# Attention and two mixture layers: the second layer's turns nested, its last blocks taken by output rows, GpSimd in one scatter loop

## What is computed

```python
logits = x @ w_gate + modality_bias[modality_id]
e_idx = np.argmax(logits, axis=1)
gate_w = softmax(logits)[np.arange(N), e_idx]
for e in range(E):
    mask = e_idx == e
    if not mask.any():
        continue
    h = np.maximum(x[mask] @ w1[e], 0.0)
    out[mask] = gate_w[mask, None] * (h @ w2[e])
```

## Time and profile before

| what | value |
|---|---|
| median of 3 runs | 1515.71 us (1514.54 to 1515.93) |
| the profiled execution's own time | 1515.54 us |
| its span | 1514.0 us |
| its mean granted clock of TensorE | 0.993 |

### The profile page before, as it was taken

How to read it: one execution, slowest core, us unless ns; L and a number is a source line. 1 busy time by engine, 2 the same in 40 slices (tenths; PEclk the granted TensorE clock), 3 DMA queues, 4 the chain that set the end, 5 groups by cost and what they waited for, 6 DMA issues and landing times.

```text
span 1514.0 us, 34658 instructions
## 1 busy us (share of the span) xinstructions
PE 1468.2 (97%) x11861; PEld 1292.1 (85%) x11861; DVE 1011.9 (67%) x2377; ACT 773.6 (51%) x1544; POOL 401.1 (26%) x379
## 2 busy tenths in 40 slices
PE   8999999999999999999899999999999999999994
PEld 7888978789888888788799999998888888888884
DVE  7989977999789998987666666665333333333331
ACT  6676767776677767665344444444333332333331
POOL 4133312334123424212322222224121221221211
PEclk9999999999999999999999999999999999999997
DMA  5311030212202020201533354323211111111110
GB/s 119 98 33 62 28 99 28 65 42 62 79 31 65 28 86 28 85 30 36 170 109 130 129 201 131 104 95 109 73 43 43 44 69 41 42 54 46 42 50 21
DMA packets 58018, 107.86 MB, mean 71 GB/s; under 512 B 18007, under 2 KB 32354, under 8 KB 57884
## 3 DMA queue, kind: packets, MB, share of 16 engines
q0 software_dynamic: 18464, 58.68, 11.1%
q1 hardware_dynamic: 39420, 47.48, 11.1%
HBM read 75.63 MB, written 32.04 MB: 71 GB/s over the span
## 4 chain that ended last, share of the span: by engine, by line
PE 81%; DVE 5%; issue 5%; DMA 4%; ACT 1%; POOL 1%; SPq 0%; POOLq 0%; ACTq 0%; DVEq 0%
PE pO L1436 23%; PE pS L1684 11%; PE pO L1696 10%; PE pS L1644 9%; PE pO L1627 9%; PE pS L1425 6%; PE pO L1698 5%; PE pM L1684 3%; DVE AH L1091 3%; DMA raw<-in_v_dram 2%; DMA token_rows<-xrow,dest 1%; PE pT L1675 1%; PE pT L1574 1%; PE pO L1445 1%; POOL token_rows L527 1%
## 5 line engine op out<-in xcount | busy, mean ns | idle before, releaser
L1093 DVE TENSOR_TENSOR AL<-A,AH 128x512 fp32r<-128x512 f32 (+1 forms) x400 | 314.4, 786 | 13.7
L1436 PE MATMUL pO<-AH,VH 64*128 64x512 f32 (+1 forms) x1520 | 306.7, 384 | 9.2 <-DVE xT L998 7.2
L1436 PE MATMUL pO<-AL,VH 64*128 64x512 f32 (+1 forms) x1520 | 305.4, 382 | 0.0
L1436 PE MATMUL pO<-AH,VL 64*128 64x512 f32 (+1 forms) x1520 | 305.1, 382 | 0.0
L709 ACT ACTIVATE R<-pS 128x512 f32<-128x512 f32 (+1 forms) x400 | 213.5, 588 | 150.4 <-PE pS L1425 134.8
L1091 DVE CAST AH<-A 128x512 fp32r<-128x512 f32 (+1 forms) x400 | 231.7, 579 | 39.8 <-ACT A L718 39.4
L718 ACT ACTIVATE A<-R 128x512 f32<-128x512 f32 (+1 forms) x400 | 229.8, 624 | 19.8 <-DVE AL L1093 19.4
L1696 PE MATMUL pO<-VL,AH 128*128 128x512 f32 x640 | 232.4, 399 | 0.0
L1351 DVE SCALAR_TENSOR_TENSOR AL<-pS,AH 128x512 fp32r<-128x512 f32 x120 | 83.0, 692 | 180.8 <-ACT AH L877 179.3
L1436 PEld LDWEIGHTS pO<-AH,VH 64*128 64x128 f32 x1520 | 154.2, 184 | 34.4 <-issue 12.6
L1698 PE MATMUL pO<-VL,AL 128*128 128x256 f32 x640 | 179.5, 280 | 0.0
(11 more groups left out here) (241 smaller groups left out, 2477.5 us busy)
## 6 DMA issues: line engine op xcount, KB each, us to landing
raw<-in_w_dram POOLq DMA_DIRECT2D x22, 1024.0 KB
A<-token_rows SPq DMA_DIRECT2D x21, 536.0 KB
uT<-in_u_dram SPq DMA_DIRECT2D x16, 512.0 KB
xin<-token_rows SPq DMA_DIRECT2D x24, 268.0 KB
raw<-in_v_dram SPq DMA_DIRECT2D x4, 1152.0 KB, 5.8
A<-in_w2t_dram POOLq DMA_DIRECT2D x8, 512.0 KB
raw<-in_v_dram SPq DMA_DIRECT2D x4, 768.0 KB, 8.1
raw<-in_z_dram SPq DMA_DIRECT2D x8, 368.0 KB
```

The costliest lines, as they stand in the source:

```text
L1093: v_.tensor_tensor(AL[k % NBUF][:, 0:n], A[k % NA][:, 0:n], AH[k % NBUF][:, 0:n].bitcast(F32), ALU.subtract).then_inc(al_ready, 1)
L1436: last = t_.matmul(pO[:, (KD * r + d) * QW:(KD * r + d) * QW + n], vv[rows, vo + k * D + d * P:vo + k * D + (d + 1) * P], a[k % NBUF][rows ...
```

## The change

On TensorE, ScalarE and VectorE the walk over the turns becomes a nest: `turns(at + 1, hi)` stands inside `If(hi < total)` of `turns(at, lo)`, so that behind the last tile one branch leaves all of it. `total` is loaded once by VectorE and TensorE ahead of it. GpSimd has one loop over tiles 1 to `total` with nothing but `scatter_out` in phase 1, and loads one entry of `cum` in place of nine; the work ahead for turns from 1 on goes to VectorE (remainders, `next_low`) and SyncE (the two loads of weights, `load_weights_behind`), both behind `If(hi < total)`. On TensorE `layer1` of block 7 goes ahead of `layer2` of block 4, and blocks 5, 6 and 7 of `layer2` are added row block by row block: all three for s = 0, then for s = 1, and so on (`layer2_last`). In tile 0 the second transpose stands between s = 1 and s = 2.

```diff
+                    def load_weights_behind(turn_):
+
+                        sp.wait_ge(wl_ready, WP * turn_ + 2 * WP)
+                        sp.sem_inc(sp_passed, 1)
+                        e = sp.value_load(order[0:1, turn_ + 2:turn_ + 3], min_val=0, max_val=2 * E - 1)
+                        sp.dma_start(stage1, w1[ds(e, 1), :, :].rearrange("o (k p) f -> p (o k) f", p=P)).then_inc(w1_loaded, 16)
+                        sp.dma_start(stage2, w2[ds(e, 1), :, :].rearrange("o (f p) d -> p (o f) d", p=P)).then_inc(w2_loaded, 16)
...
+                        if ph == 1 and at > 0:
+                            with sp.If(hi < total):
+                                load_weights_behind(at + E)
...
-            for ph in range(2):
-                q = PH[ph]
-                if ph == 1:
-                    next_weights(E, 0, True)
-                    scatter_out(0)
-                pool.wait_ge(cum_ready, ph + 1)
-
-                ends = [pool.value_load(cum[0:1, ph, i:i + 1], min_val=0, max_val=64) for i in range(E + 1)]
-                total = ends[E]
...
-                    turn_ = at + ph * E
-
-                    def ahead():
-                        if ph == 0:
-                            if at + 2 < E:
-                                wait(gcols_made, at + 1)
-                                load_w2t(at + 2)
-                            next_weights(turn_, at % 2, False)
-                        else:
-                            with pool.If(hi < total):
-                                next_weights(turn_, at % 2, True)
-
...
-                            if turn_ != E:
-                                with pool.If(t == lo):
-                                    ahead()
-                            if ph == 1:
-                                scatter_out(t)
-                    if turn_ != E:
-                        with pool.Else():
+            def scatter_rows(t):
...
+            with pool.If(total > 0):
+                scatter_rows(total)
+            next_weights(E, 0, True)
+            scatter_out(0)
+            pool.wait_ge(cum_ready, 2)
+            total = pool.value_load(cum[0:1, 1, E:E + 1], min_val=0, max_val=64)
+            with pool.If(total > 1):
+                with pool.Fori(1, total) as t:
+                    scatter_out(t)
...
-                lo = 1
-                for at in range(E):
+                def turns(at, lo):
+
                     hi = end_of(act, 1, at)
                     turn_, h = at + E, at % 2
...
-                    lo = hi
+                    if at + 1 < E:
+                        with act.If(hi < total):
+                            turns(at + 1, hi)
+
+                turns(0, 1)
                 act.wait_ge(q.stored, STORED + 16 * SUB2 * total)
...
+                total = dve.value_load(cum[0:1, 1, E:E + 1], min_val=0, max_val=64)
+                def turns(at, lo):
+
                     hi = end_of(dve, 1, at)
+
+                    def weights_ahead():
+
+                        with dve.If(hi < total):
+                            next_low(at + E + 1, 1 - at % 2)
...
+                            if at > 0:
+                                with dve.If(t == lo):
+                                    weights_ahead()
...
-                    lo = hi
+                    if at > 0:
+                        with dve.Else():
+                            weights_ahead()
+                    if at + 1 < E:
+                        with dve.If(hi < total):
+                            turns(at + 1, hi)
+
+                turns(0, 1)
...
+                def row_sums(h, f, s):
+
+                    rows = slice(s * P, (s + 1) * P)
+                    t_.matmul(pO[:, s * QW:(s + 1) * QW].rearrange("p (m d) -> p m d", m=2), AH[f][:, rows], w2hl[h][:, :, f, 0:D],
+                              start=(f == 0), stop=(f == NF - 1), skip_group_check=True)
+                    return t_.matmul(pO[:, s * QW:s * QW + D], AL[f][:, rows], w2h[h][:, f, 0:D],
+                                     start=False, stop=(f == NF - 1), skip_group_check=True)
+
                 def layer2(t, h, f):
 
                     pe.wait_ge(q.h_split, NF * t + NF + f + 1)
                     if f == 0:
                         pe.wait_ge(q.y_out, t + 1)
                     for s in range(SUB2):
-                        rows = slice(s * P, (s + 1) * P)
-                        t_.matmul(pO[:, s * QW:(s + 1) * QW].rearrange("p (m d) -> p m d", m=2), AH[f][:, rows], w2hl[h][:, :, f, 0:D],
-                                  start=(f == 0), stop=(f == NF - 1), skip_group_check=True)
-                        last = t_.matmul(pO[:, s * QW:s * QW + D], AL[f][:, rows], w2h[h][:, f, 0:D],
-                                         start=False, stop=(f == NF - 1), skip_group_check=True)
-                        if f == NF - 1:
-                            last.then_inc(q.y_made, 1)
-                    if f < NF - 1:
-                        last.then_inc(q.h_used, 1)
+                        last = row_sums(h, f, s)
+                    last.then_inc(q.h_used, 1)
+
+                def layer2_last(t, h, between=None):
+
+                    for s in range(SUB2):
+                        for f in range(NF - 3, NF):
+                            if s == 0:
+                                pe.wait_ge(q.h_split, NF * t + NF + f + 1)
+                            last = row_sums(h, f, s)
+                            if s == SUB2 - 1 and f < NF - 1:
+                                last.then_inc(q.h_used, 1)
+                        last.then_inc(q.y_made, 1)
+                        if s == 1 and between is not None:
+                            between()
...
-                for f in range(3, NF):
+                for f in range(3, NF - 1):
                     layer2(0, 0, f - 3)
                     layer1(0, 0, 0, f, hring_lead)
+                layer1(0, 0, 0, NF - 1, hring_lead)
+                layer2(0, 0, 4)
                 pe.wait_ge(q.h_split, NF + 6)
                 transpose_half(1, 0, pT)
-                layer2(0, 0, 5)
-                layer2(0, 0, 6)
-                transpose_half(1, 1, pT)
-                layer2(0, 0, 7)
+                layer2_last(0, 0, lambda: transpose_half(1, 1, pT))
                 pe.wait_ge(cum_ready, 2)
-                lo = 1
-                for at in range(E):
+                total = pe.value_load(cum[0:1, 1, E:E + 1], min_val=0, max_val=64)
+
+                def turns(at, lo):
+
                     hi = end_of(pe, 1, at)
                     h = at % 2
                     with pe.If(lo < hi):
@@ -1747,12 +1784,14 @@
                             transpose_half(t + 1, 1, pT)
                             layer2(t, h, 3)
                             layer1(t, par, h, 6, hring)
+                            layer1(t, par, h, 7, hring)
                             layer2(t, h, 4)
-                            layer1(t, par, h, 7, hring)
-                            layer2(t, h, 5)
-                            layer2(t, h, 6)
-                            layer2(t, h, 7)
-                    lo = hi
+                            layer2_last(t, h)
+                    if at + 1 < E:
+                        with pe.If(hi < total):
+                            turns(at + 1, hi)
+
+                turns(0, 1)
```

More of the change, by code:

```diff
@@ L586, in scatter_out @@
                                           bounds_check=N - 1, oob_is_err=False).then_inc(PH[1].stored, 16)
-            for ph in range(2):
-                q = PH[ph]
-                if ph == 1:
-                    next_weights(E, 0, True)
-                    scatter_out(0)
-                pool.wait_ge(cum_ready, ph + 1)
-                ends = [pool.value_load(cum[0:1, ph, i:i + 1], min_val=0, max_val=64) for i in range(E + 1)]
-                total = ends[E]
-                if ph == 0:
[L598 to L602, removed]
-                for at in range(E):
-                    lo, hi = 1 if at + ph * E == E else ends[at], ends[at + 1]
-                    turn_ = at + ph * E
-                    def ahead():
-                        if ph == 0:
-                            if at + 2 < E:
-                                wait(gcols_made, at + 1)
-                                load_w2t(at + 2)
-                            next_weights(turn_, at % 2, False)
-                        else:
-                            with pool.If(hi < total):
-                                next_weights(turn_, at % 2, True)
[L617 to L624, removed]
-                            if turn_ != E:
-                                with pool.If(t == lo):
-                                    ahead()
-                            if ph == 1:
-                                scatter_out(t)
-                    if turn_ != E:
-                        with pool.Else():
-                            ahead()
[L633 to L638, removed]
@@ new lines, in scatter_rows @@
+            def scatter_rows(t):
```

(27 more changed lines are left out.)

## The result

The changed kernel took 1507.49 us (median of 4 runs, 1503.43 to 1508.98) against 1515.82 us for the kernel before: a ratio of 0.9943, 95% interval 0.9922 to 0.9963. Measured again it was 1509.15 against 1515.96, a ratio of 0.9960 (0.9946 to 0.9973). So it is faster by some 7 to 8 us; the forecast was 8.5.

A forecast was written before the change was run, and what follows sets the result against it. TensorE bounds the kernel until the last matmul, then GpSimd's stops and DRAIN. DRAIN start 1498.43 + 6.87 + 0.25 barrier + 1.5 outside the span gives 1507.1, so 1507.2 us for the median; range 1503.0 to 1513.2.

The forecast's parts named there:

- The end is a walk over empty turns and then GpSimd's DRAIN: Behind the last matmul: GpSimd's three stops over empty turns go, so its DRAIN starts 8.5 us sooner, at 1498.43.
- The last scatters, 2.1 us: End of the last tile: row blocks become ready 1.05 us apart, so GpSimd's last scatter ends 2.1 us sooner, at 1498.83.
- The DRAIN as a cost of its own: GpSimd's DRAIN at the end keeps its recorded length of 6.87 us wherever it starts.
- The tied DRAIN: Rival: the end of GpSimd's DRAIN stays 12.9 us behind the last scatter's end, giving 1513.1 us; chance 0.2.
- The short DRAIN: Rival: GpSimd's final DRAIN becomes short and ScalarE's wait for stored rows sets the end, 1503.1 us; chance 0.12.
- Moved weight work, loads of `total`: nothing: Weight work moved to VectorE and SyncE, and register loads on VectorE and TensorE, change the time by nothing.
- Block 7, no stall: TensorE ahead of `layer2` of block 7: 1.88 us needed, 2.1 us covered, 0.2 left; rival of a stall, chance 0.05.
- Tile 0 and 1, 0.4 us less: Second transpose moves 0.7 us forward and `load_x` of tile 2 is issued sooner: 0.4 us taken as gain.
- The new order costs nothing in the tiles: TensorE's reordered blocks in each tile: matmuls and their sizes stay as they are, no cost counted.

The follow-up runs named there:

- two of three parts alone: Against the kernel before: TensorE's new block order alone, 1514.51 us, ratio 1.0004; nested turns on TensorE, ScalarE and VectorE alone, 1514.03 us, ratio 0.9997.

## Why the prediction was right, and where not

- *The end is a walk over empty turns and then GpSimd's DRAIN.* Right. The three stops are gone and the DRAIN starts behind the last scatter, in effect: it was forecast to run 6.87 us from there and ran 6.78. The span's end was forecast at M + 11.3 (1505.55 - 1494.23) and stands at M + 11.19.
- *The last scatters, 2.1 us.* Right: M + 6.29 to M + 4.17, and 1.28 us apart as counted.
- *The DRAIN as a cost of its own.* Right for this change, and for a reason that I hadn't: it depends on what GpSimd did before, which the change leaves alone. That it would keep its length was taken from one recorded DRAIN, and was in so far luck. The tied DRAIN is refuted by its end at 6.8 us behind the last scatter, where it had stood 12.9 us behind. The short DRAIN didn't come here, but its place was seen rightly: once the DRAIN is made short, ScalarE's wait is what is left, and the time is 1503.3 where the rival had 1503.1.
- *Moved weight work, loads of `total`: nothing.* Right; the page shows the same number of instructions on each engine, and TensorE is full over the turn change.
- *Block 7, no stall.* Right, with 0.6 us to spare where I counted 0.2: the remainder took 1.52 us and not 1.60, and 0.28 us for the hand-over turned out not to be needed in front.
- *Tile 0 and 1, 0.4 us less.* Wrong. `load_x` of tile 2 was issued some 0.5 us sooner against the second layer's start and TensorE came sooner too, but the rows didn't land sooner: the wait went from 0.9 to 1.3 us. The transposes of tile 2 start 32.0 to 32.5 us behind the first matmul of `layer1` with the new order and 31.9 to 32.6 with the old, no difference.
- *The new order costs nothing in the tiles.* Wrong by 0.4 us, a term that I had at zero. It is exact in all kernels: 431.06 or 431.07 us with the old order (four kernels), 431.45 to 431.47 with the new (ten executions), 0.02 us in each of 18 tiles. TensorE shows no gap in either, so it is in the spacing of matmuls. The traces show where: the last twelve pairs of `layer2` in a tile (blocks 5 to 7) take 4.07 us from the first start to the last in block order and 4.11 in row block order, the same in every kernel of either kind. That is 0.04 us a tile, 0.7 in all, of which the rest of the tile gives back 0.3. Why the pairs stand further apart is open.

The two misses together are 0.8 us and the rest came out as summed. The second, larger measurement (6.8 us less) fits that: 8.2 from the span's end less 0.4 for the tiles is 7.8.

## What to carry to other kernels

Read the stretch behind the last matmul by the sequencers' rows, not by busy shares: here 13 of 19 us held no busy engine and were branches, what I read as code loads, and one DRAIN. Ends that stand one behind the other must all be moved: two of three parts alone gave nothing that the time could tell. Where GpSimd has issued many DMAs, give it a DRAIN at a place where it waits anyway, near the end; one early DRAIN did next to nothing, one in each tile took over 5 us off the end.

## What the runs showed of the hardware

- A DRAIN of GpSimd at the end took 6.78 to 6.87 us behind 206 indirect DMAs and 42 others, 6.3 behind 76 indirect ones, and 1.5 to 1.8 behind 4, where it ended 0.5 to 0.6 us behind their last packet. In mid-program, behind 130 and the 42 others, it was 5.1 to 5.3. On the other engines it took 0.01 to 0.09 us. The Trainium skill, in "VectorE: DVE Perf Modes" under The DRAIN you can't avoid, gives about 12 ns on all five engines for the DRAINs of the preamble and postamble, which the runtime puts around a kernel. Those at L65 are the program's own: with `no_gpsimd_drain=True` GpSimd's was gone. For SyncE and ScalarE the rows come out alike (13 and 8 ns); to GpSimd's DRAIN the page's figure doesn't carry over.
- A taken branch over a loop body cost TensorE 2.3 to 3.5 us. GpSimd stopped three times for 2.2 to 2.4 us, once for each two empty turns.
- The first matmul of the second layer's first `layer1` stands at 1029.3 to 1034.5 us over the fourteen traces, and at 1034.5 and 1032.3 in two of the same kernel. From there to tile 2 it is 31.9 to 32.6 us, and from tile 2 to M each order repeats within 0.02 us. A change of 1 us can be read from a trace by distances from a fixed instruction, and not from the times.
